# VectorE's jumped-over general path as a loop over tiles, and the order of a fused attention and mixer kernel's first steps

## The reference, cut to what matters

```python
# attention
scores = q @ k.T / sqrt(64)
keep = (pos_k < n_sink) | ((pos_q - pos_k >= 0) & (pos_q - pos_k < window))
scores = where(keep, scores, -1e9)
a = exp(scores - max(scores)); a = a / (sum(a) + 1e-9)
x = a @ v                                  # -> (2, 768, 512)
# gated spatial unit
h = relu(x @ w_in); u, v = split(h)        # w_in 512 x 1024
v_n = (v - mean(v)) / sqrt(var(v) + 1e-6)
x = (u * (w_spatial @ v_n + b_spatial)) @ w_out
# mixer
h = relu(x.T @ w_tok1) @ w_tok2
u = x + h.T
out = u + relu(u @ w_ch1) @ w_ch2
```

## Time and profile before

| | us |
|---|---|
| median of 3 runs (508.4 to 509.59) | 509.5 |
| the profiled execution's own time | 508.11 |
| its span, first to last instruction | 506.3 |
| TensorE busy | 495.1 (98%) |
| VectorE busy | 211.2 (42%) |
| ScalarE busy | 173.1 (34%) |
| GpSimd busy | 154.9 (31%) |

### The profile page before, as it was taken

The page is one execution under the profiler, slowest core; times in us unless marked ns, Lnnn a source line. Parts: engine busy times, 40 slices in busy tenths (PEclk is TensorE's granted clock), DMA queues, the critical chain, the costliest instruction groups (busy, mean ns, idle before and its releaser), DMA issues.

```text
span 506.3 us, 7183 instructions
## 1 busy us (share of the span) xinstructions
PE 495.1 (98%) x2678; PEld 438.1 (87%) x2678; DVE 211.2 (42%) x528; ACT 173.1 (34%) x365; POOL 154.9 (31%) x163
## 2 busy tenths in 40 slices
PE   6899999999999999999999999999999999999997
PEld 4788999999999999999888898888888888888885
DVE  5577876777576317754222242122131131211212
ACT  5677766666665242112432232110010010010010
POOL 3544443533323488602205057970000000000000
PEclk9599999999999999999999999999999999999999
DMA  7454323432221234300202013420020000200002
GB/s 239 151 174 162 105 88 97 141 109 88 81 65 46 65 86 129 88 1 5 74 0 79 6 53 97 141 64 0 1 84 1 0 1 0 74 10 0 1 0 83
DMA packets 19190, 34.04 MB, mean 67 GB/s; under 512 B 2256, under 2 KB 4560, under 8 KB 19152
## 3 DMA queue, kind: packets, MB, share of 16 engines
q1 hardware_dynamic: 19008, 33.55, 21.1%
q10 hardware_dynamic: 144, 0.00, 0.0%
HBM read 30.39 MB, written 3.15 MB: 66 GB/s over the span
## 4 chain that ended last, share of the span: by engine, by line
PE 92%; DMA 2%; POOL 2%; DVE 1%; issue 1%; ACT 1%; SPq 0%; DVEq 0%; ACTq 0%
PE bank L955 24%; PE bank L956 24%; PE bank L957 24%; PE bank L1028 7%; PE bank L994 4%; PE bank L970 2%; PE bank L971 2%; PE bank L1036 2%; PE bank L1010 1%; PE bank L1194 1%; DMA stage<-w_in 1%; DMA stage<-w_sp 1%; POOL wsp_lo L538 1%; DMA par_i<-params 1%; POOL vn_lo L549 1%
## 5 line engine op out<-in xcount | busy, mean ns | idle before, releaser
L944 DVE SCALAR_TENSOR_TENSOR hch_lo<-bank,hch_hi 128x512 fp32r<-128x512 f32 x36 | 24.9, 691 | 153.8 <-ACT hch_hi L732 153.8
L732 ACT ACTIVATE hch_hi<-bank 128x512 fp32r<-128x512 f32 x36 | 21.5, 598 | 169.0 <-PE bank L957 169.0
L613 ACT ACTIVATE probs<-masked,small 128x288 f32<-128x288 f32 (+1 forms) x96 | 48.8, 509 | 39.2 <-DVE small L784 38.5
L957 PE MATMUL bank<-up_hi,wc_lo 128*128 128x512 f32 x144 | 56.0, 389 | 0.0
L956 PE MATMUL bank<-up_lo,wc_hi 128*128 128x512 f32 x144 | 56.0, 389 | 0.0
L955 PE MATMUL bank<-hch_hi,wc_hi 128*128 128x512 f32 x144 | 56.0, 389 | 0.0
L956 PE MATMUL bank<-hch_lo,wc_hi 128*128 128x512 f32 x144 | 56.0, 389 | 0.0
L955 PE MATMUL bank<-up_hi,wc_hi 128*128 128x512 f32 x144 | 56.0, 389 | 0.0
L957 PE MATMUL bank<-hch_hi,wc_lo 128*128 128x512 f32 x144 | 56.0, 389 | 0.0
L784 DVE CUSTOM_DVE_ANT_0 masked<-bank,masks 128x288 f32<-128x288 f32 (+1 forms) x96 | 40.8, 427 | 36.3 <-PE bank L971 32.0
L516 POOL TENSOR_TENSOR k_lo<-k_raw,k_hi 128x512 fp32r<-128x512 f32 x24 | 30.7, 1280 | 72.1 <-ACT k_hi L581 72.1
(11 more groups left out here) (123 smaller groups left out, 1029.1 us busy)
## 6 DMA issues: line engine op xcount, KB each, us to landing
k_raw<-kT SPq DMA_DIRECT2D x24, 256.0 KB, 2.9
q_raw<-qT SPq DMA_DIRECT2D x24, 256.0 KB, 3.0
stage<-w_c SPq DMA_DIRECT2D x24, 256.0 KB, 2.7
v_sl<-vL SPq DMA_DIRECT2D x12, 264.0 KB, 2.8
outT<-out_sb SPq DMA_DIRECT2D x12, 256.0 KB, 2.6
stage<-w_sp SPq DMA_DIRECT2D x12, 192.0 KB, 2.6
stage<-w_in SPq DMA_DIRECT2D x8, 256.0 KB, 3.5
stage<-w_out SPq DMA_DIRECT2D x4, 256.0 KB, 3.0
```

Of the source, the lines that this page charges most:

```text
L613: act.activation(probs[:, n % N_PROB, 0:w], masked[:, n % N_MASKED, 0:w], ACT.Exp, bias=least[:, n % 8:n % 8 + 1], scale=-1.0).then_inc(ex ...
L732: act.activation(hch_hi[:, u[2] % N_HCH, :], bank[:, :], ACT.Relu).then_inc(hi_ready, 1)
L944: dve.scalar_tensor_tensor(out=hch_lo[:, f % N_HCH, :], in0=bank[:, :], scalar=0.0, in1=hch_hi[:, f % N_HCH, :], op0=ALU.max, op1=ALU.subt ...
L957: return pe.matmul(out, a_lo, b_hi, start=False, stop=last, skip_group_check=skip)
```

## The change

- VectorE's body of the general path becomes a loop over 96 tiles with 15 operations in it, in place of a loop over 16 heads with 72. The tile's offset is now held in two columns of `g_small` and stepped by three more operations; two memsets ahead of the loop clear them. The other engines' bodies are as before.
- `load_qk(3)`, `stage_in(3)`, the sink values and `stage_in(4)` are issued by SyncE ahead of its flag, in this order.
- `q_high(1)` on ScalarE goes from step 1 to ahead of step 0; `q_low(1)` on VectorE from step 2 to step 1.
- `later_keeps` goes from step 1 to 3, `general_flag` from step 2 to 5, ScalarE's masks of the second tile from step 2 to 4.
- `sinks_gather(g)` goes from step 4g + 4 to 4g + 3.

```diff
-                for g in range(2, N_GROUP + 4):
-                    if 3 <= g < N_GROUP:
+                for g in range(3, N_GROUP + 4):
+                    if 4 <= g < N_GROUP:
                         load_qk(g)
...
-                    if 3 <= g + 1 < EARLY:
+                    if 5 <= g + 1 < EARLY:
                         stage_in(g + 1)
-                    if g == 3:
-                        load_sink_values(0)
...
             load_v(1)
+            load_qk(3)
+            stage_in(3)
+            load_sink_values(0)
+            stage_in(4)
...
             k_high(1)
+            q_high(1)
...
-                if n == 2:
+                if n == 4:
                     mask_by_act((MASK_SECOND, second_keep, P), (MASK_SECOND + P + SINKS, diag_keep, P))
...
-                if n % 4 == 0 and n // 4 - 1 in sink_n:
-                    sinks_gather(n // 4 - 1)
+                if n % 4 == 3 and n // 4 in sink_n:
+                    sinks_gather(n // 4)
...
-                if n % 4 == 1 and n // 4 + 1 < N_GROUP:
+                if n % 4 == 1 and 2 <= n // 4 + 1 < N_GROUP:
                     q_high(n // 4 + 1)
...
-            def general_head(g):
-                for i in range(NT):
-                    n = [0]
-                    at_ = g * (NT * G_X) + i * G_X
...
+            def general_tile(t):
...
+                then(dve.tensor_scalar(g_keep, g_rel, tile_at, par[:, 1:2], ALU.add, ALU.is_lt))
...
+                then(dve.tensor_scalar(tile_at, tile_at, float(P), None, ALU.add))
+                then(dve.scalar_tensor_tensor(out=tile_at, in0=tile_at, scalar=float(S), in1=tile_at,
+                                              op0=ALU.is_lt, op1=ALU.mult))
+                then(dve.tensor_scalar(minus_at, tile_at, -1.0, None, ALU.mult))
...
                         dve.wait_ge(g_const, 32)
-                        with dve.Fori(0, HEADS) as g:
-                            general_head(g)
+                        dve.memset(tile_at, 0.0).then_inc(g_zero, 1)
+                        dve.memset(minus_at, 0.0).then_inc(g_zero, 1)
+                        dve.wait_ge(g_zero, 2)
+                        with dve.Fori(0, HEADS * NT) as t:
+                            general_tile(t)
...
-                if n % 4 == 2 and n // 4 + 1 < N_GROUP:
+                if n == 1:
+                    q_low(1)
+                if n % 4 == 2 and 2 <= n // 4 + 1 < N_GROUP:
                     q_low(n // 4 + 1)
-                if n == 1:
+                if n == 3:
                     later_keeps()
-                if n == 2:
+                if n == 5:
                     general_flag()
```

More of the change, by code:

```diff
@@ L253, in build @@
         g_x = at("g_x", C_VN + S * 10, [D])
-        g_small = at("g_small", C_VN + S * 10 + D, [4])
+        g_small = at("g_small", C_VN + S * 10 + D, [6])
+        tile_at, minus_at = g_small[:, 4:5], g_small[:, 5:6]
         xg = nc.dram_tensor("xg", [HEADS, NT, P, D], F32).ap()
@@ L317, in build @@
         s_general = sem("general_flag_ready")
+        g_zero = sem("g_first_tile")
         g_const, g_load, g_stored = sem("g_const_loaded"), sem("g_operands_loaded"), sem("g_stored")
@@ L394, in load_flag @@
             return eng.value_load(general[0:1, 0:1], min_val=0, max_val=1)
-        G_KEEP, G_LEAST, G_SUM, G_X = 4, 8, 10, 12
+        G_LEAST, G_X = 8, 15
         SPATIAL_AT = {N_HEAD + 4 + 2 * k: EARLY + k for k in range(NT)}
@@ new lines, in general_tile, with then @@
+            def general_tile(t):
+                n = [0]
+                def then(ins):
+                    n[0] += 1
+                    ins.then_inc(g_step, 1)
+                    dve.wait_ge(g_step, t * G_X + n[0])
+                then(dve.tensor_scalar(g_keep, g_rel, tile_at, par[:, 1:2], ALU.add, ALU.is_lt))
+                then(dve.scalar_tensor_tensor(out=g_keep, in0=g_rel, scalar=minus_at, in1=g_keep, op0=ALU.is_ge, op1=ALU.mult))
+                then(dve.scalar_tensor_tensor(out=g_keep, in0=g_key, scalar=par[:, 0:1], in1=g_keep,
+                                              op0=ALU.is_lt, op1=ALU.max))
+                then(dve.tensor_scalar(g_hole, g_keep, -MASKED, MASKED, ALU.mult, ALU.add))
+                dve.wait_ge(g_scored, t + 1)
+                for c in range(2):
+                    cols = slice(HALF * c, HALF * c + HALF)
+                    then(dve.scalar_tensor_tensor(out=g_masked[:, cols], in0=first_bank[c][:, 0:HALF],
+                                                  scalar=-float(D) ** -0.5, in1=g_keep[:, cols],
+                                                  op0=ALU.mult, op1=ALU.mult))
+                then(dve.tensor_tensor(g_masked, g_masked, g_hole, ALU.add))
+                then(dve.tensor_reduce(g_small[:, 0:1], g_masked, mybir.AxisListType.X, ALU.min))
+                assert n[0] == G_LEAST
+                then(dve.tensor_scalar(tile_at, tile_at, float(P), None, ALU.add))
+                then(dve.scalar_tensor_tensor(out=tile_at, in0=tile_at, scalar=float(S), in1=tile_at,
+                                              op0=ALU.is_lt, op1=ALU.mult))
+                then(dve.tensor_scalar(minus_at, tile_at, -1.0, None, ALU.mult))
+                dve.wait_ge(g_valued, t + 1)
+                then(dve.tensor_scalar(g_small[:, 1:2], first_bank[0][:, D:D + 1], EPS_SUM, None, ALU.add))
+                then(dve.reciprocal(g_small[:, 2:3], g_small[:, 1:2]))
+                dve.wait_ge(g_stored, t * 16 + 16)
+                then(dve.tensor_scalar(g_x[:, :], first_bank[0][:, 0:D], g_small[:, 2:3], None, ALU.mult))
+                then(dve.tensor_copy(g_small[:, 3:4], g_small[:, 2:3]))
+                assert n[0] == G_X
```

## The result

The changed kernel takes 505.75 us (median of 5 runs, 505.49 to 506.2); the kernel before took 509.5 in the same job (508.19 to 510.23). The ratio, which is that of the means of the runs, is 0.9934 with a 95% interval of 0.9920 to 0.9948, so it is faster by 0.66% (the two medians alone give 0.74%).

The account below looks back on a forecast made before the run. The chain before w_in's first product at 29.96 us was taken as the bound, nearly all TensorE after it. The stall's 2.03 us plus an earlier clock return gave 2.4, from 509.5 to 507.1 us, range 505.8 to 509.3.

Parts of the forecast that it names:

- part 1: VectorE's jump over its skipped general body: shorter body removes the stall, mask of score 8 starts 2.03 us sooner.
- second rival: VectorE's jump: the stall stays, since body length is not its cause; only 0.1 us gained, 509.4; chance 0.13.
- Parts 2 to 4: First steps: second group's queries sooner, second tile's masks later on ScalarE, flag and later masks later on VectorE; each worth zero.
- part 4: Flag and later masks moved back on VectorE: zero, as the flag's 0.4 us delay for TensorE is covered by 1.3.
- Part 5: SyncE's load queue: fifth group's keys issued at 19.0, not 18.17, covered by 0.4 or more; slow transfer loses up to 0.6.
- Part 6: Sink gathers one step sooner on ScalarE: 0 to 0.2 us gained, 0.1 taken as nothing.
- case (b): Steps 8 to 14: full clock returns near 21.5 us, not 25, so score 14 starts 2.4 us sooner; chance 0.48.

Follow-up runs that it names:

- e1: The kernel before with VectorE's loop over tiles as its only edit, all orders old: 506.33 us against 509.06, ratio 0.9953.
- e3: The changed kernel with 130 never-run memsets added in VectorE's skipped block: 508.03 us against 509.06 for the kernel before, ratio 0.9988.
- e9: The changed kernel with 40 or 80 never-run memsets in VectorE's skipped block: 506.72 and 506.03 us, one run each, against 510.83 for the kernel before.
- e6: The changed kernel with second group's queries, second tile's masks, later masks and flag at their old steps: 506.31 us, ratio 0.9936 (changed kernel 0.9934).
- e7: The changed kernel with SyncE's old load order, behind the flag: 509.49 us, ratio 1.0002 to the kernel before.
- e10: The kernel before with SyncE's new load order as its only edit: 508.31 us in one run, against 510.83 for the kernel before.
- e2: The changed kernel with VectorE's old body (loop over heads), all changes of order kept: 507.98 us against 509.06 for the kernel before, ratio 0.9978.
- e4: The changed kernel with 9 idle TensorE products before the transpose of head 3 and 4 ahead of the flag: 506.68 us, ratio 0.9957 to the kernel before.

## Why the prediction was right, and where it was not

**The stall (part 1): right.** Taken as 2.03 us, measured as 1.72: mask of score 8 at 17.34 instead of 19.06. The jump itself, taken as 0.5 us, took 0.61, covered as I said. Of the 0.31 between, 0.17 is w_in's first piece, which landed that much later in this execution, as score 8 shows (16.36 for 16.18); 0.14 is the modelled end of the score matmul, from which I took the start. e1, e3 and e9 show the cause, and the second rival (the stall stays, as by the Trainium skill's figure) is out. One premise was false: TensorE's branch does not go over the longest body. In the built program its loop has 98 instructions, ScalarE's 32, and VectorE's old one, with 165, is the longest of the three, so that their jumps are short shows nothing about one as long as VectorE's.

**Parts 2 to 4: right as a sum, incomplete as separate claims.** Score 4 at 9.37 (9.35 forecast), exps 3 still behind w_in's piece, the third group's queries 1.70 us under GpSimd's lock and through at 16.30, the flag late and read in time by TensorE. e6 shows the zero. But part 4's zero named only TensorE, VectorE and ScalarE as readers; for SyncE I priced the new order alone. e7 shows the missing sentence: with the old order of the loads behind the late flag, 4.1 us are lost against the changed kernel and 2.7 against e1. And at step 9 ScalarE's masks of the third tile and its queries came into the chain, which I had not named as what is late next: TensorE waited 0.36 for them before score 12.

**Part 5: right.** The fifth group's keys were issued at 19.26 (19.0 forecast), and no wait for a transfer stands in the chain between 20 and 30 us. I had not seen that the load order also shortens VectorE's stall (e10).

**Part 6: the step that failed.** I put a gather one step sooner at 0 to 0.2 us and took 0.1. It brought 0.6 by the 200th matmul, of which 0.15 was given back where the spatial products wait for GpSimd's v_n; 0.45 in the span. I had read the waits of matmuls alone. TensorE's weight loads had three more waits at the same line, 0.9 us together, put down to "issue".

**The clock: case (b) came true, but not by its rule.** The clock fell at 13.4 us and came back at 20.2 (21.5 forecast), so after 6.8 us, where before it took 13.7. Steps 12 to 14 then ran at the full clock, and score 14 started at 24.23, 1.98 sooner; I had 2.4, because VectorE's 1.72 is what there was and ScalarE set the pace. In the span the smaller clock term and the larger gather term cancel: 2.36 measured, 2.4 forecast. That is luck.

My rule for the rise, that it follows TensorE's unbroken run, does not hold. Stretches at the low clock, up to its rise, in the changed kernel, in e1 and in e2:

```profile
16.40:20.10 3.70, 3.70 (x16) 3.67 (x17) 2.55 (x12) 2.80 (x9) 2.04 (x2) 0.50 0.31 94
```

```profile
16.60:22.90 6.30, 6.30 (x28) 6.25 (x29) 4.21 (x18) 5.11 (x14) 3.46 (x3) 0.50 0.64 208
```

```profile
20.40:28.80 8.40, 8.37 (x37) 8.26 (x38) 4.82 (x17) 6.36 (x15) 3.84 (x3) 0.50 0.59 166
```

TensorE is all but without a gap in all three, and the clock stays low for 3.7 us more in one and for 8.4 in another. What sets its return stays open. It mattered little here: e1, whose clock came back only at 23.0, was 1.76 us ahead of before at score 16, where the changed kernel was 1.98.

**From one execution to the median: too small by 1.35 us.** I subtracted the trace's difference from the median. The 36 timed executions of the kernel before in two of the jobs have a mean granted clock of 0.983 in 13 (median 509.78), of 0.986 or 0.987 in 22 (medians 508.52 and 508.78), and 0.980 in one (510.2). Worked out from the span, 0.983 is 17 us of low clock and 0.986 is 14. The profiled execution was one of the second kind. The five of the changed kernel have 0.989 to 0.993: 7 to 11 us. So, as I read it, the change also took away the longer kinds, about 1.1 us each time they came, and with them most of the spread (2.0 us before, 0.7 after). The median held that gain and the pair of traces did not. This is argued from runs of other jobs: the clocks of the five runs of before beside the changed kernel are not on record. With 3 or 5 runs of before, part of the 1.35 us may be scatter; the 36 have a median of 509.1.

## What to carry to other kernels

A block that is never run still costs where it makes a jump long or puts its target far into the program: here 129 instructions fewer in the loop of VectorE's skipped body, with nothing else changed in what is run, were worth 0.47% (e1), and it was a step and not a slope. A flag may be set late only if everything that the reader's queue holds behind it is not needed soon, so the flag and the loads have to be moved together. And when the waits of TensorE are read, those of its weight loads belong to them.

## What the runs showed of the hardware that was not expected

- VectorE's jump: 0.61 us from the branch to the next instruction with its target at the 90th, 130th or 170th instruction (e9), 2.9 to 3.5 us with it at the 217th or 220th (15.69 to 18.55 in e3). SyncE's took 0.51 us and ScalarE's 0.17 in the kernel before; TensorE's took 0.43 in the changed kernel. All three jump over fewer instructions than VectorE did before.
- The length of that gap went with the order of the loads: 3.50 us before, 2.88 with the fourth group's transfers issued sooner (e10), 2.86 in e2 and e3.
- The same program has low stretches of the clock of different length in different executions (14 and 17 us before, 7 to 11 us after, worked out from the mean granted clock), and executions with the longer one took 0.9 to 1.3 us more (medians 508.52 and 509.78 before; e2's 507.76 at a mean granted clock of 0.986 or 0.987 and 508.63 at 0.983).
- Keeping TensorE busy through its waits did not save time: in the profiled execution the clock fell at 21.3 us and not at 13.4, in the stage where TensorE has no gaps (e4).
- TensorE without a gap at the low clock got the full clock back after 3.7 us in the changed kernel and not for 8.4 us in e2.
